# Returning the softmax sums: two wide blocks and three small products in place of three narrow blocks and two transposes

## The chip, the cores and the metric

The kernel runs on one core of a Trainium2 chip. The metric is the device time of one execution in microseconds (us). Lower is better.

## The reference

An attention over 32 heads (batch 4 x 8 heads, 1152 keys, head size 64) is followed by two mixture-of-experts layers over the 2304 resulting rows. The attention pools the queries in pairs, so that there are 576 of them for each head:

```python
q_pool = q.reshape(B, H, S // 2, 2, D).mean(axis=3)
scores = scale * np.matmul(q_pool, k.transpose(0, 1, 3, 2))
scores = scores - np.max(scores, axis=-1, keepdims=True)
attn = np.exp(scores)
attn = attn / (np.sum(attn, axis=-1, keepdims=True) + 1e-09)
return np.matmul(attn, v).astype(np.float32)
```

The change concerns `np.sum(attn, axis=-1)`: one number for each of the 576 queries of a head. The two layers behind it (rows of 512 numbers, 8 experts with hidden size 1024, one expert for each row, the first with a skip decision) are the same before and after.

## The kernel before

**Stages.** The first half of the time is attention, head by head; then the rows, sorted by expert, go through the two layers in tiles of 128. While the attention of a head runs, the numbers by which its rows will be routed are computed too (`back_logits`, `divide`).

**The attention of a head.** Scores stand transposed: keys on the partitions (9 tiles of 128, index `t`), the 576 queries in two halves of 288 columns. For each `t` TensorE makes the scores (L566 and L571, two parts of one product), ScalarE takes the exponent into `P` (L850), and GpSimd adds the nine tiles of `P` up into `Acc`, 128 x 576 (L443, L446). TensorE also makes blocks of scores of the next head (`prior`, L556), which VectorE reduces to row maxima (L1037), and transposes keys and queries of the heads to come (`trans_k`, `trans_qh`, `trans_ql`; all transposes have the line L504).

**The way back of a head.** When head `h` runs, head `h - 1` is finished off. `weighted` (L587) multiplies by the values: the output, 64 partitions for each half of the queries, lies in a PSUM bank as two column blocks of 64, one for each half. `sums` (L600) then multiplies `Acc` by a block of ones, which adds up its 128 partitions; since every column of the stationary block is ones, each block of output partitions holds the same sums. ScalarE copies the outputs to `OT` (L866) and the sums to `ST` (L870). `back_values` transposes `OT` in three pieces of 96 queries, `back_sums` brings the sums of `ST` to the same 96 partitions, `back_logits` multiplies `OT` by the routing weights (L622), and VectorE's `divide` adds 1e-9, takes the reciprocals (L1053) and multiplies.

**Order.** TensorE's order is written out by hand in `body(h)`: for every `t` the scores, two `prior` blocks and then what is listed under `if t == ...`. The values' third group and the sums stand at t = 4, `back_values` and `back_sums` at t = 5, `back_logits` at t = 6. Each engine works through its own list; semaphores join them. `sums` waits for `acc_step` (GpSimd), `back_values` for `ot_out` and `st_out` (ScalarE), `divide` for `out_done` (the last of L622). `body` runs for h = -2 to 32; heads are 0 to 31. PSUM bank `TR` (7) takes transposes and the sums, bank `OB` (6) the outputs, the routing logits and the ranks. In GpSimd's list, some rows are scattered between heads (L460).

The f32 products have two records each in the trace, one for each pass; transposes have one.

Of the kernel before, what the change touches and what calls it, by code (L numbers as in the profile page):

```python
# [5 lines left out]
def attention_moe_moe(nc, q, k, v, w_skip, w_gate1, w1a, w2a, w_gate2, w_ogate, w1b, w2b, out):  # L6
# [11 lines left out]
    ALU, ACT, AX = mybir.AluOpType, mybir.ActivationFunctionType, mybir.AxisListType  # L18
    ds = bass.ds
    PN = 128  # L20


    B, H, S, D = q.shape
    NH = B * H
    SQ = S // 2
    HQ = SQ // 2
# [8 lines left out]
    OP = 96  # L35
    OJ = HQ // OP
# [28 lines left out]
    with ctx:  # L65
        def sb(name, shape, dt=f32):
            return ctx.enter_context(nc.sbuf_tensor(name, shape, dt))

        def sem(name):
            return ctx.enter_context(nc.semaphore(name))  # L70
# [36 lines left out]
        Acc = view["acc"]  # L107
# [2 lines left out]
        QHT = [at(f"QHT{u}", M_K + 4 * (5 * S + u * SQ), [PN, SQ], f32r) for u in range(3)]  # L110
        QLT = [at(f"QLT{u}", M_K + 4 * (5 * S + (3 + u) * SQ), [D + 1, SQ], f32r) for u in range(2)]
        OT = sb("OT", [PN, HQ])
        SG = 3
        SW = SQ // SG
        SR = 32 * (SG - 1) + 1
        SJ = SW // OP
        ST = sb("ST", [SR, SW])
        mx3 = sb("mx3", [PN, QT, NB])
        den = sb("den", [OP, 2 * OJ])
        rden = sb("rden", [OP, 2 * OJ])  # L120
# [4 lines left out]
        ident = sb("ident", [PN, PN])  # L125
        ones = sb("ones", [PN, 64])
# [96 lines left out]

        PS = ctx.enter_context(nc.psum_tensor("PS", [PN, 8, 512], f32))
        MXB, SB, OB, TR = 0, 2, 6, 7
        LOG, RANK, SUMS = 0, 192, 288
        HB, XTB, YB, X1B, LB, RKB = 0, 2, 3, 4, 5, 6


# [17 lines left out]
        sum_done, st_out = sem("sum_done"), sem("st_out")  # L247
        out_done = sem("out_done")
        norm = sem("norm")
# [5 lines left out]
        def wait(eng, s, val):  # L255

            if val > 0:
                eng.wait_ge(s, val)
# [17 lines left out]
        def has(g):  # L276
            return 0 <= g < NH
# [224 lines left out]
        def _(pe):  # L502
            def transpose(o, i, n=PN):
                return nc.tensor.transpose(o, i, ident[0:n, 0:n])  # L504

            def keep_busy(n, bank=OB):

                for _ in range(n):
                    transpose(PS[:, bank, 0:PN], ident[:, :])
# [83 lines left out]
            def sums(g):  # L593

                pe.wait_ge(acc_step, ACCS * (g + 1))
                if has(g + 3):
                    pe.wait_ge(qht_out, 2 * (g + 3) + 2)
                wait(pe, norm, HEAD_NORM * (g - 1) + 4)
                for r in range(SG):
                    last = nc.tensor.matmul(PS[32 * r:32 * r + 32, TR, 0:SW], ones[:, 0:32],  # L600
                                            Acc[g % 2][:, r * SW:(r + 1) * SW], start=True, stop=True)
                last.then_inc(sum_done, 1)

            def back_values(g):

                pe.wait_ge(ot_out, g + 1)
                pe.wait_ge(st_out, g + 1)
                for j in range(OJ):
                    transpose(PS[0:OP, TR, j * PN:(j + 1) * PN], OT[:, j * OP:(j + 1) * OP])

            def back_sums(g):

                for n in range(SJ):
                    transpose(PS[0:OP, OB, SUMS + n * SR:SUMS + (n + 1) * SR], ST[:, n * OP:(n + 1) * OP], SR)

            def back_logits(g):

                if g == 0:
                    pe.wait_ge(wrh_in, 16 * 8)
                for j in range(OJ):  # L620
                    o = LOG + j * 2 * NL
                    last = nc.tensor.matmul(PS[0:OP, OB, o:o + 2 * NL], OT[:, j * OP:(j + 1) * OP],  # L622
                                            wrh[:, g % H].rearrange("p a n -> p (a n)"), start=True, stop=True)
                last.then_inc(out_done, 1)
# [23 lines left out]
            def body(h):  # L648

                now, after, before = has(h), has(h + 1), has(h - 1)  # L650
                blocks = iter(range(NBLK))
                for t in range(KT):
                    if t == 3 and has(h + 2):
                        trans_qh(h + 2, 0)
                    if now:
                        scores(h, t, 0)
                    if after and t < 7:
                        prior(h + 1, next(blocks))
                    if after and t < 7 and h <= 0:
                        keep_busy(1)  # L660
                    if now:
                        scores(h, t, 1)
                    if after and t < 7:
                        prior(h + 1, next(blocks))
                    if after and t < 7 and h <= 0:
                        keep_busy(2 if h < 0 else 1)
                    if t == 0:
                        if has(h + 2):
                            trans_k(h + 2, 0)
                            if h == FIRST:  # L670
                                keep_busy(14)
                        if before:
                            weighted(h - 1, 0)
                    if t == 1 and has(h + 2):
                        trans_k(h + 2, 1)
                        if h == FIRST:
                            keep_busy(5)
                    if t == 2 and before:
                        weighted(h - 1, 1)
                    if t == 3 and has(h + 2):  # L680
                        if h == FIRST:
                            keep_busy(5)
                        trans_qh(h + 2, 1)
                        if h == FIRST:
                            keep_busy(4)
                    if t == 4:
                        if before:
                            weighted(h - 1, 2)
                            sums(h - 1)
                        if after:  # L690
                            prior(h + 1, next(blocks))
                    if t == 5 and before:
                        back_values(h - 1)
                        back_sums(h - 1)
                    if t == 6 and h - 2 in RANKS_IN:
                        ranks_of_batch(RANKS_IN.index(h - 2))
                    if t == 6 and before:
                        back_logits(h - 1)
                    if t == 7 and after:
                        trans_ql(h + 1, 0)  # L700
                        trans_ql(h + 1, 1)
# [73 lines left out]
            for m in range(2):  # L775
                pe.wait_ge(tables[m], 1)
                trans_x(m, 0)
                start = 0
                for e in range(E):
# [15 lines left out]
                    start = end  # L795
# [15 lines left out]
        def _(act):  # L811
# [55 lines left out]

            def s_out(g):
                act.wait_ge(sum_done, g + 1)
                nc.scalar.copy(ST[:, :], PS[0:SR, TR, 0:SW]).then_inc(st_out, 1)  # L870

            def route_exps(b):

# [55 lines left out]
            for m in range(2):  # L929
# [12 lines left out]
                start = 0  # L942
                for e in range(E):
# [27 lines left out]
                    start = end  # L971
# [5 lines left out]
        def _(dve):  # L977
            vec = nc.vector
# [66 lines left out]
            def divide(g):  # L1045

                T = PS[0:OP, TR, 0:OJ * PN].rearrange("p (j a d) -> p j a d", j=OJ, a=2)
                dve.wait_ge(out_done, g + 1)
                total = PS[0:OP, OB, SUMS:SUMS + SJ * SR].rearrange("p (n k) -> p n k", n=SJ)[:, :, 0:SR:32]
                vec.tensor_scalar(den.rearrange("p (r n) -> p r n", n=SJ), total.rearrange("p n r -> p r n"),  # L1050
                                  1e-9, None, ALU.add).then_inc(norm, 1)
                dve.wait_ge(norm, HEAD_NORM * g + 1)
                vec.reciprocal(rden[:, :], den[:, :]).then_inc(norm, 1)  # L1053
                dve.wait_ge(norm, HEAD_NORM * g + 2)
                b, c = g // H, (g % H) * D
                by = rden[:, :].rearrange("p (a j) -> p j a", a=2).unsqueeze(3)
                vec.tensor_tensor(tmpL[:, :, :, :], PS[0:OP, OB, LOG:LOG + OJ * 2 * NL]
                                  .rearrange("p (j a n) -> p j a n", j=OJ, a=2),
                                  by.broadcast_to([OP, OJ, 2, NL]), ALU.mult).then_inc(norm, 1)
                if b >= 2 and g % H == 0:  # L1060
                    dve.wait_ge(rt_scat[b % 2], 16 * TB * (b // 2))
                vec.tensor_tensor(xrow[b % 2][:, :, c:c + D].rearrange("p (a j) d -> p j a d", a=2), T,
                                  by.broadcast_to([OP, OJ, 2, D]), ALU.mult).then_inc(norm, 1)
                dve.wait_ge(norm, HEAD_NORM * g + 3)
                Lb = L[:, b * TB:(b + 1) * TB, :].rearrange("p (a j) n -> p j a n", a=2)
                vec.tensor_tensor(Lb, Lb, tmpL[:, :, :, :], ALU.add).then_inc(norm, 1)
# [197 lines left out]
            for m in range(2):  # L1264
# [12 lines left out]
                start = 0  # L1277
                for e in range(E):
# [28 lines left out]
                    start = end  # L1307
# [28 lines left out]
```

## Time and profile before

| | |
|---|---|
| median of three runs | 1139.82 us (1138.76 to 1144.27) |
| the profiled execution | 1139.82 us |
| its span, first to last instruction | 1138.1 us |
| TensorE matmuls busy | 1093.4 us, 96% |
| VectorE, ScalarE, GpSimd busy | 740.7, 531.8, 452.8 us |
| sums, L600 | 192 matmuls, 338 ns each in the median |
| transposes of `ST` | 64 matmuls, 220 ns each in the median |
| logits, L622 | 192 matmuls, 248 ns each in the median |

How to read it: matmuls overlap, the next starting before the end of the one before, so that their durations don't add up. The distance from start to start is what one of them takes of the engine's time. "PEld" is the load of the stationary operand, which has a record of its own. Shapes such as 128*96 128x50 mean: a stationary operand of 128 partitions and 96 columns, a moving operand of 128 partitions and 50 columns; the moving operand is named first behind the arrow.

### The profile page before, as it was taken

To read this page: it belongs to the slowest core of one execution; us is meant where nothing else is said; L and a number is where in the kernel's file an instruction comes from. 1 tells how busy PE (TensorE), PEld (TensorE's weight loads), DVE (VectorE), ACT (ScalarE), POOL (GpSimd) and SP (SyncE) were. 2 spreads that over 40 slices of the span, in tenths; PEclk is the share of its full clock that TensorE was granted. 3 is DMA by queue.
4 is the path that set the end of the run, shared out by engine and by line. 5 is a ranking of instruction groups with operands and counts; after the bars stand their busy time and mean duration, and the time that the engine had idled before them with its cause. 6 is when DMAs were issued, how large, how long until landed. Compare 5 with 4: busy or idle time off the path is not lost.

```text
span 1138.1 us, 22000 instructions
## 1 busy us (share of the span) xinstructions
PE 1093.4 (96%) x7757; PEld 916.7 (81%) x7757; DVE 740.7 (65%) x1706; ACT 531.8 (47%) x945; POOL 452.8 (40%) x339
## 2 busy tenths in 40 slices
PE   7999999999999999999779999999699999999996
PEld 6777777777777777777578999999589999999995
DVE  7767767887778777785436777676445655555641
ACT  3566655555655555564124444444143434353420
POOL 0768877677877788677600000000000000001000
PEclk8999999999999999999899999999799999999998
DMA  5272225223322233211649014447384281241100
GB/s 130 66 229 74 63 74 147 74 69 92 102 64 73 74 94 93 76 33 39 220 159 366 28 37 177 170 173 273 134 322 132 111 317 54 58 156 37 46 10 15
DMA packets 74397, 132.59 MB, mean 117 GB/s; under 512 B 11040, under 2 KB 29472, under 8 KB 74320
## 3 DMA queue, kind: packets, MB, share of 16 engines
q10 hardware_dynamic: 26240, 69.22, 16.8%
q1 hardware_dynamic: 43424, 50.58, 16.6%
q0 software_dynamic: 4656, 11.79, 3.0%
q8 instruction: 45, 0.74, 0.3%
q14 instruction: 32, 0.26, 0.1%
HBM read 106.12 MB, written 19.24 MB: 110 GB/s over the span
## 4 chain that ended last, share of the span: by engine, by line
PE 86%; DVE 5%; issue 2%; DMA 2%; POOL 2%; ACTq 1%; ACT 1%; SPq 0%; DVEq 0%; POOLq 0%
PE PS L734 20%; PE PS L587 13%; PE PS L556 9%; PE PS L504 8%; PE PS L566 7%; PE PS L571 7%; PE PS L751 6%; PE PS L747 6%; PE PS L748 6%; DVE W2L L1142 2%; PE PS L622 1%; PE PS L600 1%; PE PS L766 1%; POOL arena_a L446 1%; DMA moe<-xs 1%
## 5 line engine op out<-in xcount | busy, mean ns | idle before, releaser
L446 POOL TENSOR_TENSOR arena_a<-arena_a,arena_p 128x576 f32<-128x576 f32 x224 | 332.9, 1486 | 86.6 <-ACT arena_p L850 63.8
L1037 DVE TENSOR_REDUCE mx<-PS 128x1 f32<-128x384 f32 (+1 forms) x480 | 246.8, 551 | 110.6 <-PE PS L556 106.7
L734 PE MATMUL PS<-moe,W 128*128 128x128 f32 x2432 | 281.3, 277 | 1.6 <-ACT moe L936 1.6
L734 PEld LDWEIGHTS PS<-moe,W 128*128 128x128 f32 x2432 | 278.4, 193 | 4.0 <-ACT moe L936 2.2
L850 ACT ACTIVATE arena_p<-PS 128x576 f32<-128x576 f32 x288 | 187.7, 653 | 135.7 <-PE PS L571 135.1
L566 PE MATMUL PS<-QHT,KA 128*128 128x288 f32 x576 | 187.1, 329 | 0.0
L556 PE MATMUL PS<-KA,QHT 128*128 128x384 f32 (+1 forms) x480 | 176.1, 368 | 1.8 <-DVE mx L1037 1.8
L571 PE MATMUL PS<-QLT,KB 65*128 65x288 f32 x576 | 171.3, 301 | 0.3 <-ACT QLT L861 0.3
L822 ACT CAST W2H<-W2R 128x1024 fp32r<-128x1024 f32 x148 | 144.3, 1048 | 52.7 <-PE PS L751 39.7
L1142 DVE TENSOR_TENSOR W2L<-W2R,W2H 128x1024 fp32r<-128x1024 f32 x144 | 166.5, 1219 | 1.4 <-ACT W2H L822 1.4
L587 PE MATMUL PS<-arena_p,arena_a 128*64 128x288 f32 x1152 | 160.5, 414 | 0.0
L494 POOL DMA_INDIRECT out<-moe,oidx x23 | 22.8, 990 | 294.6 <-DVE moe L1302 294.6
L956 ACT ACTIVATE hTh<-PS 128x512 fp32r<-128x512 f32 x76 | 45.2, 596 | 190.5 <-PE PS L734 190.5
L747 PE MATMUL PS<-W2H,hTh 128*128 128x512 f32 x304 | 123.7, 407 | 1.3 <-ACT hTh L956 1.3
L566 PEld LDWEIGHTS PS<-QHT,KA 128*128 128x128 f32 x576 | 109.3, 190 | 16.8 <-issue 14.3
L748 PE MATMUL PS<-W2L,hTh 128*128 128x512 f32 x304 | 119.1, 392 | 0.0
L587 PEld LDWEIGHTS PS<-arena_p,arena_a 128*64 128x64 f32 x1152 | 74.3, 136 | 55.2 <-issue 16.9
L571 PEld LDWEIGHTS PS<-QLT,KB 65*128 65x128 f32 x576 | 109.1, 189 | 5.7 <-issue 5.7
L477 POOL DMA_INDIRECT xs<-moe,tpu x16 | 18.0, 1123 | 225.3 <-DVE tpu L1261 225.3
L556 PEld LDWEIGHTS PS<-KA,QHT 128*128 128x128 f32 (+1 forms) x480 | 86.4, 180 | 21.9 <-DVE mx L1037 9.5
L751 PE MATMUL PS<-W2H,hTl 128*128 128x512 f32 x304 | 82.7, 394 | 3.9 <-DVE hTl L1221 3.9
L504 PE MATMUL PS<-ident,arena_a 128*128 128x128 f32 (+2 forms) x480 | 81.7, 279 | 4.2 <-DVE KA L1023 2.1
(174 smaller groups left out, 1138.8 us busy)
## 6 DMA issues: line engine op xcount, KB each, us to landing
W<-in_moe_w ACTq DMA_DIRECT2D x16, 2048.0 KB, 15.0
W2R<-in_moe_w ACTq DMA_DIRECT2D x16, 2048.0 KB, 9.8
moe<-xs SPq DMA_DIRECT2D x40, 258.0 KB, 2.7
arena_a<-in_k SPq DMA_DIRECT2D x32, 288.0 KB, 2.9
arena_a<-in_v SPq DMA_DIRECT2D x32, 288.0 KB, 2.8
KB<-KA SPq DMA_DIRECT2D x32, 288.0 KB, 3.1
arena_a<-in_q SPq DMA_DIRECT2D x32, 256.0 KB, 3.2
xs<-padrow SPq DMA_DIRECT2D x8, 258.0 KB, 3.3
```

Of the source, the lines that this page charges most:

```text
L446: nc.gpsimd.tensor_tensor(Acc[u], Acc[u], P[u][:, t, :], ALU.add).then_inc(acc_step, 1)
L504: return nc.tensor.transpose(o, i, ident[0:n, 0:n])
L556: nc.tensor.matmul(PS[0:n, MXB + b % 2, 0:KB_], QHT[g % 3][:, t * PN:t * PN + n], KA[g % 3][:, c * KB_:(c + 1) * KB_], start=True, stop=Tr ...
L566: nc.tensor.matmul(o, KA[g % 3][:, t * PN:(t + 1) * PN], QHT[g % 3][:, cols], start=True, stop=False)
L571: last = nc.tensor.matmul(o, KB[u][:, t * PN:(t + 1) * PN], QLT[u][:, cols], start=False, stop=True)
L587: last = nc.tensor.matmul(PS[64 * half:64 * half + D, OB, 0:HQ], Vt[u][:, t, :], P[u][:, t, half * HQ:(half + 1) * HQ], start=(t == 0), st ...
L734: last = nc.tensor.matmul(PS[:, HB + f // 4, (f % 4) * PN:(f % 4 + 1) * PN], W1[s][:, d, f * PN:(f + 1) * PN], xT[:, d, :], start=(d == 0) ...
L747: nc.tensor.matmul(PS[:, YB, 0:DM], hTh[:, f, :], W2H[s][:, f, :], start=(f == 0), stop=False)
L748: nc.tensor.matmul(PS[:, YB, 0:DM], hTh[:, f, :], W2L[s][:, f, :], start=False, stop=False)
L850: nc.scalar.activation(P[u][:, t, :].rearrange("p (a c) -> p a c", a=2), PS[:, b:b + 2, 0:HQ], ACT.Exp, scale=SCALE).then_inc(exp_done, 1)
L1037: vec.reduce_max(mx3[0:n, t, c:c + 1], PS[0:n, MXB + b % 2, 0:KB_], AX.X).then_inc(pr_max, 1)
L1142: ins = vec.tensor_tensor(W2L[s][:, f, :], W2R[s][:, f, :], W2H[s][:, f, :].bitcast(f32), ALU.subtract)
```

## The change

The sums are made by two products with a stationary block of 64 ones and 288 moving columns each, one for each half of the queries, in place of three with a block of 32 ones and 192 columns. So `ST` holds one half's sums in its first 64 partitions and the other's in partition 64 (65 partitions, 288 columns; before 65 and 192, with the three thirds in partitions 0, 32 and 64).

To bring them to the 96 partitions, `ST` is no longer transposed (two transposes of 96 columns, 65 moving columns each, into bank `OB`). It is the stationary operand of three products of 96 columns, and the moving operand is two columns of the identity, 0 and 64, which pick the two partitions: six numbers for each partition, in bank `TR` behind the transposed outputs. These stand in TensorE's list at t = 6, ahead of `back_logits`, and no longer at t = 5. ScalarE copies 288 columns in place of 192, and `divide` reads six adjoining columns and the order of pieces and halves in `den` and `rden` is turned round.

```diff
-        SG = 3
-        SW = SQ // SG
-        SR = 32 * (SG - 1) + 1
-        SJ = SW // OP
-        ST = sb("ST", [SR, SW])
+        SR = D + 1
+        ST = sb("ST", [SR, HQ])
...
-                for r in range(SG):
-                    last = nc.tensor.matmul(PS[32 * r:32 * r + 32, TR, 0:SW], ones[:, 0:32],
-                                            Acc[g % 2][:, r * SW:(r + 1) * SW], start=True, stop=True)
+                for half in range(2):
+                    last = nc.tensor.matmul(PS[64 * half:64 * half + 64, TR, 0:HQ], ones[:, 0:64],
+                                            Acc[g % 2][:, half * HQ:(half + 1) * HQ], start=True, stop=True)
...
-                for n in range(SJ):
-                    transpose(PS[0:OP, OB, SUMS + n * SR:SUMS + (n + 1) * SR], ST[:, n * OP:(n + 1) * OP], SR)
+                for j in range(OJ):
+                    o = OJ * PN + 2 * j
+                    nc.tensor.matmul(PS[0:OP, TR, o:o + 2], ST[:, j * OP:(j + 1) * OP],
+                                     ident[0:SR, 0:SR:SR - 1], start=True, stop=True)
...
                     if t == 5 and before:
                         back_values(h - 1)
-                        back_sums(h - 1)
...
                     if t == 6 and before:
+                        back_sums(h - 1)
                         back_logits(h - 1)
...
-                nc.scalar.copy(ST[:, :], PS[0:SR, TR, 0:SW]).then_inc(st_out, 1)
+                nc.scalar.copy(ST[:, :], PS[0:SR, TR, 0:HQ]).then_inc(st_out, 1)
...
-                total = PS[0:OP, OB, SUMS:SUMS + SJ * SR].rearrange("p (n k) -> p n k", n=SJ)[:, :, 0:SR:32]
-                vec.tensor_scalar(den.rearrange("p (r n) -> p r n", n=SJ), total.rearrange("p n r -> p r n"),
-                                  1e-9, None, ALU.add).then_inc(norm, 1)
+                both = PS[0:OP, TR, OJ * PN:OJ * (PN + 2)]
+                vec.tensor_scalar(den[:, :], both, 1e-9, None, ALU.add).then_inc(norm, 1)
...
-                by = rden[:, :].rearrange("p (a j) -> p j a", a=2).unsqueeze(3)
+                by = rden[:, :].rearrange("p (j a) -> p j a", a=2).unsqueeze(3)
```

## Rows read from the trace of the kernel before

**Rows 1.** The page: span, and each engine's busy time, share and instructions.

```profile
span 1138.1 us, 22000 instructions
...
PE 1093.4 (96%) x7757; PEld 916.7 (81%) x7757; DVE 740.7 (65%) x1706; ACT 531.8 (47%) x945; POOL 452.8 (40%) x339
```

**Rows 2.** Busy time by stretch (us; instructions), granted TensorE clock, DMA share, GB/s.

```profile
37.00:300.00 263.00, 262.80 (x1894) 199.02 (x1894) 191.98 (x434) 156.46 (x310) 202.55 (x136) 1.00 0.36 99
...
316.50:532.00 215.50, 215.50 (x1558) 163.44 (x1558) 166.47 (x380) 122.90 (x246) 159.13 (x110) 1.00 0.27 71
532.00:553.00 21.00, 19.87 (x155) 14.08 (x156) 4.92 (x14) 9.11 (x18) 18.84 (x15) 1.00 0.28 86
553.00:577.60 24.60, 14.31 (x103) 13.22 (x97) 10.96 (x53) 1.39 (x4) 9.36 (x10) 0.72 0.73 266
```

**Rows 3.** Timeline, TensorE, end of one head's values to the next transposes.

```profile
314.23 0.66 PE L587 MATMUL PS<-arena_p,arena_a 128*64 128x288 f32 x4
...
314.47 0.41 PE L587 MATMUL PS<-arena_p,arena_a 128*64 128x288 f32 x2
314.81 0.53 PE L600 MATMUL PS<-arena_a,ones 128*32 128x192 f32 x6
315.27 0.44 PE L556 MATMUL PS<-KA,QHT 128*128 128x384 f32 x1
...
316.59 0.49 PE L504 MATMUL PS<-ident,OT 128*96 128x128 f32 x3
...
317.22 0.29 PE L571 MATMUL PS<-QLT,KB 65*128 65x288 f32 x1
...
319.05 0.71 PE L504 MATMUL PS<-ident,arena_a 128*65 128x128 f32 x5
...
319.73 0.30 PE L571 MATMUL PS<-QLT,KB 65*128 65x288 f32 x1
```

**Rows 4.** Timeline, TensorE: inside one group of logits products (L622).

```profile
318.10 0.50 PE L622 MATMUL PS<-wrh,OT 128*96 128x50 f32 x4
...
318.27 0.33 PE L622 MATMUL PS<-wrh,OT 128*96 128x50 f32 x2
```

**Rows 5.** Timeline, TensorE: 16-column products and the shortest steps, second half.

```profile
622.17 0.60 PE L766 MATMUL PS<-wr,moe 128*128 128x16 f32 x4
622.62 0.48 PE L747 MATMUL PS<-W2H,hTh 128*128 128x512 f32 x1
...
625.47 0.18 PE L772 MATMUL PS<-tRb,trib 128*128 128x16 bf16 x1
625.51 0.17 PE L773 MATMUL PS<-Raccb,onesb 128*128 128x16 bf16 x1
```

**Rows 6.** Weight loads by form (line, stationary shape, count, busy us, mean ns).

```profile
L622 PEld LDWEIGHTS PS<-wrh,OT 128*96 128x96 f32 x192 | 21.2, 166 | 0.3
...
L504 PEld LDWEIGHTS PS<-ident,OT 128*96 128x96 f32 x96 | 11.4, 125 | 1.8 <-issue 0.9
L504 PEld LDWEIGHTS PS<-ident,ST 65*96 65x96 f32 x64 | 7.6, 127 | 0.0
```

**Rows 7.** Timeline, VectorE and ScalarE around the same head.

```profile
321.08 1.02 DVE L1037 TENSOR_REDUCE mx<-PS 128x1 f32<-128x384 f32 x2 [0.34 <-PE PS L556]
...
314.93 0.40 ACT L866 COPY OT<-PS 128x288 f32<-128x288 f32 x1 [1.14 <-PE PS L587]
...
316.46 0.65 ACT L850 ACTIVATE arena_p<-PS 128x576 f32<-128x576 f32 x1 [0.74 <-PE PS L571]
```

**Rows 8.** Timeline, GpSimd in the last two heads, then all engines after it.

```profile
532.10 6.08 POOL L446 TENSOR_TENSOR arena_a<-arena_a,arena_p 128x576 f32<-128x576 f32 x4 [1.45 <-ACT arena_p L850]
...
542.08 10.70 POOL L446 TENSOR_TENSOR arena_a<-arena_a,arena_p 128x576 f32<-128x576 f32 x7
...
552.83 0.53 PE L600 MATMUL PS<-arena_a,ones 128*32 128x192 f32 x6 [1.13 <-POOL arena_a L446]
...
553.41 0.32 ACT L870 COPY ST<-PS 65x192 f32<-65x192 f32 x1 [1.26 <-PE PS L600]
```

More of the change, by code:

```diff
@@ L225, in attention_moe_moe @@
         MXB, SB, OB, TR = 0, 2, 6, 7
-        LOG, RANK, SUMS = 0, 192, 288
+        LOG, RANK = 0, 192
         HB, XTB, YB, X1B, LB, RKB = 0, 2, 3, 4, 5, 6
```

## The prediction

> **What bounds the kernel now.** I read the page's totals first: TensorE's matmul queue is busy for 96% of the span, the next engine, VectorE, for 65% [rows 1]. An average over stages decides nothing, so the busy time by stretch came next. The edit touches only the attention stage, and there TensorE is busy for 262.80 of 263.00 us and for all of a further 215.50 us, at a granted clock of 1.00, its upper level of 2.4 GHz; VectorE, ScalarE and GpSimd each have a fifth or more of the same stretches free [rows 2]. So from 37 to 532 us a nanosecond more or less on TensorE moves everything behind it, and work on another engine counts only where TensorE waits for it. TensorE's timeline was then read step by step, from the start of one group of instructions to the start of the next: a matmul's own duration overlaps that of its neighbour and is no price [rows 3].
>
> In the last stretch before the second part this changes: from 532 to 553 us TensorE is idle for 1.1 us [rows 2]. GpSimd's timeline shows why: its additions start each without a pause behind the one before, until the last sum matmuls, which wait 1.13 us for them [rows 8]. So head 31 ends when GpSimd does, and TensorE's work of head 30's return (done while head 31 runs) is hidden.
>
> **The sums (L600).** Before, three column blocks of 32 run side by side, 192 columns each, in two passes. From the last pair of value matmuls to the matmul behind the sums is 315.27 - 314.47 = 0.80 us: 0.34 us until the sums start, 0.46 us for them [rows 3]. After, they are two column blocks of 64 with 288 columns, which is the exact form of L587. That form's pairs start 0.24 us apart (314.47 - 314.23), and a change of form costs more: 0.34 us from the last pair to the next form [rows 3]. If the sums simply go on as two more pairs of L587's form, the time is 0.24 + 0.24 + 0.34 = 0.82 us: **+0.02 us** for a head. The larger column count is paid for by one change of form less. If the border between the two groups costs a change of form in spite of equal shapes, it is 0.34 + 0.24 + 0.34 = 0.92 us: +0.12 us. I take the first, since shape and place on the array are the same. (The Trainium skill, TensorEngine Tiling (Array Packing), section Key Properties, says that changing the tiling mode drains TensorE and changing only the tile does not; by that rule it is +0.02 us, and without it +0.12 us, and the 0.10 us beyond the pair's own pace at a change of form agrees with it.)
>
> **The sums' way back, removed.** Two transposes of `ST` stood behind the three of `OT`. From the first of those to the L571 behind them is 317.22 - 316.59 = 0.63 us. The five transposes at 319.05, followed by the same L566 and L571, take 319.73 - 319.05 = 0.68 us, and their own pace is 0.11 us each (128 columns, the same as for `OT`), so three alone would take 0.68 - 2 x 0.11 = 0.46 us [rows 3]. Removed: **-0.17 us**.
>
> **The sums' way back, added.** Three f32 products, stationary `ST` 65x96, moving 2 columns. The trace has two records for each f32 product (192 of L622 for 32 heads of three), so six matmuls with six weight loads. None of this form exists before. The nearest row is L622: the same 96 stationary columns, f32, 50 moving columns; its matmuls start 0.17 us apart for two, 0.085 us each [rows 4]. With 128 stationary and only 16 moving columns (L766) the step is longer, (622.62 - 622.17) / 4 = 0.112 us [rows 5]: fewer moving columns and yet slower, so the step follows the weight load and not the moving data. The load's length goes by columns and not rows, for the transposes of 128 and of 65 rows with 96 columns take 125 and 127 ns [rows 6]. So 6 x 0.085 = **+0.51 us**. Bounds: upwards 6 x 0.112 = 0.67 us; downwards the shortest step of two small products, L772 to L773, 0.04 us [rows 5], which is also 0.085 less the 41 ns by which a transpose's weight load is shorter than L622's [rows 6]: 6 x 0.04 = 0.24 us; below that nothing at all, if the six slipped wholly under their neighbours. I take 0.085, the row with the same type and stationary columns. (The Trainium skill, TensorE: Matmul & The Clock Gate, section LDWEIGHTS (loading the stationary operand), puts a load at the column count divided by 1.2 in ns, whatever the rows: 80 ns for 96 columns, six for 0.48 us; the step of 0.085 agrees.)
>
> **What else moves.** The products stand at t = 6 instead of t = 5 and wait for nothing new there. ScalarE's copy into `ST` grows from 192 to 288 columns. The copy of 288 columns beside it takes 0.40 us against its own 0.32 us [rows 7, 8], so +0.08 us, hidden behind the 0.74 us that ScalarE then waits for scores [rows 7]; The copy of `OT` starts at 314.93 and takes 0.40 us, another 0.40 us for `ST` ends it all by about 315.8, and `back_values`, which waits for it, starts at 316.59 [rows 3, 7]. Without that cover it would be 0.08 us a head, 2.6 us in all. VectorE's `divide` can begin some 0.5 us later, behind the longer group; queued behind it are `pool_q` and the next maxima, and VectorE waits 0.34 us for TensorE before those [rows 7]; TensorE itself comes to them some 0.36 us later, so nothing is short. DMAs, GpSimd's queue and SP's are the same.
>
> **The sum.** A head: +0.02 - 0.17 + 0.51 = +0.36 us. The returns of heads 0 to 28 run inside the TensorE-bound stretch: 29 x 0.36 = 10.4 us. Head 29's is done while head 30 runs, up to the border at 532 us: its sums count (+0.02), the products behind are hidden by GpSimd, which works without a pause from 532.10 [rows 8]; head 30's is hidden likewise. Head 31's has no cover: the sums +0.12 us (from 0.53 to 0.24 + 0.41, [rows 3, 8]), the copy +0.08, the way back +0.34, together 0.5 us. In all +11.0 us. The profiled execution took 1139.82 us, of which 1138.1 are the span, and it is the median of the three runs as well: 1139.8 + 11.0 = **1150.8, say 1151 us**.
>
> **Rivals.** What can be told from no change in this kernel is about 0.5%, 5.7 us.
> - Same work, but a change of form at the border of values and sums: 30 x 0.10 = 3 us more, 1154 us. For it: L600 shows 0.34 us there now; against it: its shape differs, the new one's doesn't.
> - The new loads are priced like L766's: 29 x 6 x 0.027 = 4.7 us more, 1156 us. Against it: those have 128 columns.
> - Not slower beyond what can be measured: the six small products step at 0.04 us. Then a head costs +0.02 - 0.17 + 0.24 = +0.09 us, the total is 3 us, 1143 us. For it: the moving data are 2 columns, and L772/L773 do it; against it: those are bf16, and f32 loads hold L622 and L766 back. It decides from the point where a product steps in under 0.055 us (29 x 0.18 + 0.5 = 5.7 us).
> - The added time is absorbed by waits of TensorE in each head: only head 31's 0.5 us stays, 1140 us. Against it: 262.80 of 263.00 us busy.
> - The six products cost nothing: 29 x -0.15 us = -4.3 us, 1136 us, on the edge of faster. It needs a step of zero, which no row has.
>
> **How the numbers follow.** Main case 0.73; change of form 0.10; loads as L766's 0.04; steps of 0.04 us 0.08; absorbed 0.03; free 0.02. Slower by over 0.5% in the first three: 0.87; within 0.5% in the next two: 0.11; faster 0.02. The range must leave out no more than 2 in 10: 1146 to 1157 us holds the first three. Its lower end allows products of 0.06 us; both ends leave some 2 us for the second part, which starts 11 us later in a stretch with the granted clock at 0.72 on average [rows 2], so that the clock may rise at another point of the work. The main case's own range is 1148 to 1154 us.
>
> **What would show it.** In the changed profile: the matmul of the new way back x192, about 0.085 us from start to start, with weight loads of about 166 ns; the sums starting 0.24 us, not 0.34 us, behind the last L587 pair, and 0.82 us from there to L556; 0.46 us from the first `OT` transpose to L571; heads 0.36 us further apart than the present distance; TensorE still without idle time from 37 us to the last two heads; VectorE's wait before the next maxima not grown. The prediction is wrong if the small products step far under 0.085 us, if the border drains, or if `ST` or `den` turns up as something TensorE waits for.

## The result, and the profile after

The changed kernel takes 1151.59 us in the median of five runs (1149.71 to 1152.43), the kernel before 1140.47 us in the same measurement (1138.76 to 1144.27). The ratio is 1.0093, with a 95% interval of 1.0078 to 1.0107: slower by 11.1 us. The forecast was 11.0 us slower, 1151 us. Single executions of one kernel lie up to 5.5 us apart here, so an agreement to 0.1 us in the total says little; the steps below say more.

The totals of the page and three stretches of the changed kernel (us busy for TensorE, its weight loads, VectorE, ScalarE, GpSimd, with instructions; then granted clock, DMA share, GB/s), beside [rows 1, 2]:

```profile
span 1151.4 us, 22128 instructions
...
PE 1108.2 (96%) x7821; PEld 934.3 (81%) x7821; DVE 740.1 (64%) x1706; ACT 534.6 (46%) x945; POOL 454.2 (39%) x339
```

```profile
37.00:300.00 263.00, 262.80 (x1884) 202.41 (x1882) 189.37 (x428) 155.03 (x303) 198.95 (x134) 1.00 0.35 97
300.00:543.00 243.00, 243.00 (x1744) 187.29 (x1742) 182.26 (x417) 136.26 (x271) 177.90 (x123) 1.00 0.28 72
543.00:564.00 21.00, 20.59 (x160) 14.89 (x158) 4.47 (x14) 9.32 (x18) 18.80 (x14) 1.00 0.24 74
```

TensorE is as full as before and gets through fewer of the old instructions: in the first 263 us it does 1884 matmuls in place of 1894, although each head has two more, and every other engine is busy for a little less of the same stretch. That is what a bound engine with more to do looks like; the share of 96% did not move at all. Such a share hides short waits, though. This line of the weight loads of the changed kernel is one of them:

```profile
322.58 0.13 PEld L553 LDWEIGHTS PS<-KA,QHT 128*64 128x64 f32 x1 [0.18 <-DVE mx L1036]
```

The third `prior` block in this stretch waits for a maximum of VectorE, and its start comes 0.23 us behind the one before, where it is 0.14 us a moment earlier (321.90 to 322.04). The kernel before has the same wait at 316.36 us, so it takes nothing from the comparison.

The timeline of TensorE shows the steps. These rows answer to [rows 3, 4] (L584 is the old L587, L597 the old L600, L553 the old L556, L563 the old L566, L568 the old L571, L621 the old L622; L612 is new):

```profile
320.66 0.41 PE L584 MATMUL PS<-arena_p,arena_a 128*64 128x288 f32 x2
320.90 0.66 PE L597 MATMUL PS<-arena_a,ones 128*64 128x288 f32 x4
321.49 0.44 PE L553 MATMUL PS<-KA,QHT 128*128 128x384 f32 x1
...
322.81 0.49 PE L501 MATMUL PS<-ident,OT 128*96 128x128 f32 x3
...
323.27 0.30 PE L568 MATMUL PS<-QLT,KB 65*128 65x288 f32 x1
...
324.03 0.59 PE L612 MATMUL PS<-ident,ST 65*96 65x2 f32 x6
324.06 0.56 PE L612 MATMUL PS<-ident,ST 65*96 65x2 f32 x5
324.48 0.69 PE L621 MATMUL PS<-wrh,OT 128*96 128x50 f32 x6
324.99 0.38 PE L563 MATMUL PS<-QHT,KA 128*128 128x288 f32 x1
325.21 0.29 PE L568 MATMUL PS<-QLT,KB 65*128 65x288 f32 x1
325.34 0.29 PE L563 MATMUL PS<-QHT,KA 128*128 128x288 f32 x1
325.47 0.30 PE L568 MATMUL PS<-QLT,KB 65*128 65x288 f32 x1
```

The line at 324.06 is a closer view of the one above it: the last five of the six. They and the border to L621 are five steps of 0.085 us; the first step is 0.03 us.

The sums start 0.24 us behind the last value pair and no longer 0.34, and from that pair to L553 it is 321.49 - 320.66 = 0.83 us (before 0.80). From the first transpose of `OT` to L568 it is 0.46 us (before 0.63). From the first small product to the instruction behind the logits it is 324.99 - 324.03 = 0.96 us; the logits alone took 0.45 us before (317.97 to 318.42). So +0.03, -0.17 and +0.51: +0.37 us. The trace's median distance from one head's `OT` transposes to the next head's went from 16.53 to 16.91 us, +0.38 us.

The weight loads by form, beside [rows 6] (count, busy us, mean ns): the new load is as long as that of L621, of 128 rows, and not as short as that of a transpose of the same `ST` (127 ns in [rows 6]).

```profile
L612 PEld LDWEIGHTS PS<-ident,ST 65*96 65x96 f32 x192 | 21.0, 164 | 0.3
...
L621 PEld LDWEIGHTS PS<-wrh,OT 128*96 128x96 f32 x192 | 18.9, 165 | 0.0
...
L501 PEld LDWEIGHTS PS<-ident,OT 128*96 128x96 f32 x96 | 11.3, 125 | 1.9 <-issue 1.1
```

The last head's way back, all engines, beside [rows 8]:

```profile
564.08 0.71 PE L597 MATMUL PS<-arena_a,ones 128*64 128x288 f32 x4 [0.49 <-POOL arena_a L443]
...
564.83 0.40 ACT L869 COPY ST<-PS 65x288 f32<-65x288 f32 x1 [0.80 <-PE PS L597]
```

The last sums begin at 564.08 us and no longer at 552.83, 11.25 us later, and TensorE waits 0.49 us for GpSimd there, not 1.13. From the start of the sums to the copy it is 0.75 us in place of 0.58, and the copy takes 0.08 us more.

### The profile page after: what moved, and what is told of

Its sections match the earlier page's. It is cut to its first block, busy times and chain, and to the rows that moved or that the text cites. A ratio compares the mean times of both kernels' runs of the same rounds, so it can differ in the third digit from the quotient of the medians.

```text
span 1151.4 us, 22128 instructions
## 1 busy us (share of the span) xinstructions
PE 1108.2 (96%) x7821; PEld 934.3 (81%) x7821; DVE 740.1 (64%) x1706; ACT 534.6 (46%) x945; POOL 454.2 (39%) x339
## 4 chain that ended last, share of the span: by engine, by line
PE 87%; DVE 5%; issue 2%; DMA 2%; POOL 2%; DVEq 0%; ACT 0%; ACTq 0%; SPq 0%; POOLq 0%
PE PS L733 21%; PE PS L584 13%; PE PS L553 9%; PE PS L501 8%; PE PS L563 7%; PE PS L568 7%; PE PS L750 6%; PE PS L746 6%; PE PS L747 6%; PE PS L621 1%; DVE W2L L1140 1%; PE PS L597 1%; PE PS L765 1%; PE PS L612 1%; POOL arena_a L443 1%
## 5 line engine op out<-in xcount | busy, mean ns | idle before, releaser
L563 PE MATMUL PS<-QHT,KA 128*128 128x288 f32 x576 | 187.0, 329 | 0.0
L553 PE MATMUL PS<-KA,QHT 128*128 128x384 f32 (+1 forms) x480 | 176.2, 368 | 1.8 <-DVE mx L1036 1.8
L568 PE MATMUL PS<-QLT,KB 65*128 65x288 f32 x576 | 171.1, 301 | 0.3 <-ACT QLT L860 0.3
L584 PE MATMUL PS<-arena_p,arena_a 128*64 128x288 f32 x1152 | 160.5, 414 | 0.0
L563 PEld LDWEIGHTS PS<-QHT,KA 128*128 128x128 f32 x576 | 109.4, 190 | 17.0 <-issue 14.5
L584 PEld LDWEIGHTS PS<-arena_p,arena_a 128*64 128x64 f32 x1152 | 74.4, 136 | 55.2 <-issue 16.9
L568 PEld LDWEIGHTS PS<-QLT,KB 65*128 65x128 f32 x576 | 109.1, 189 | 6.0 <-issue 6.0
L553 PEld LDWEIGHTS PS<-KA,QHT 128*128 128x128 f32 (+1 forms) x480 | 86.4, 180 | 25.9 <-issue 13.1
```

What stands on the lines that cost most here:

```text
L553: nc.tensor.matmul(PS[0:n, MXB + b % 2, 0:KB_], QHT[g % 3][:, t * PN:t * PN + n], KA[g % 3][:, c * KB_:(c + 1) * KB_], start=True, stop=Tr ...
L563: nc.tensor.matmul(o, KA[g % 3][:, t * PN:(t + 1) * PN], QHT[g % 3][:, cols], start=True, stop=False)
L568: last = nc.tensor.matmul(o, KB[u][:, t * PN:(t + 1) * PN], QLT[u][:, cols], start=False, stop=True)
L584: last = nc.tensor.matmul(PS[64 * half:64 * half + D, OB, 0:HQ], Vt[u][:, t, :], P[u][:, t, half * HQ:(half + 1) * HQ], start=(t == 0), st ...
```

## The experiments

What each kernel took, and the median distance from head to head in its trace, which is the sharper measure: the changed kernel, e6 and e7, whose TensorE has the same list but for the moved columns, agree in it to 0.002 us. The whole times hold more than the heads. In these traces the first products with the values start anywhere from 39.5 to 42.5 us, before any sums; e3 and e9 start latest (42.47 and 42.31 us), the kernel before and the changed one at 40.38 and 40.53 us. Why is open. "Against before" is the difference from the kernel before in the same measurement.

| kernel | median us | before us | ratio, 95% interval | against before | head to head us |
|---|---|---|---|---|---|
| before | | 1140.47 | | | 16.53 |
| changed | 1151.59 | 1140.47 | 1.0093 (1.0078 to 1.0107) | +11.1 | 16.91 |
| e1_two_blocks_transposed | 1142.67 | 1139.39 | 1.0023 (1.0012 to 1.0034) | +3.3 | 16.61 |
| e2_three_blocks_products | 1144.62 | 1139.39 | 1.0043 (1.0026 to 1.0059) | +5.2 | 16.71 |
| e3_border | 1158.43 | 1139.39 | 1.0159 (1.0140 to 1.0177) | +19.0 | 17.11 |
| e4_again_96 | 1167.39 | 1139.39 | 1.0242 (1.0225 to 1.0259) | +28.0 | 17.42 |
| e5_again_72 | 1164.77 | 1141.06 | 1.0217 (1.0200 to 1.0234) | +23.7 | 17.33 |
| e6_moving_65 | 1151.12 | 1141.06 | 1.0087 (1.0071 to 1.0104) | +10.1 | 16.91 |
| e7_copy_twice | 1151.06 | 1141.06 | 1.0094 (1.0074 to 1.0114) | +10.0 | 16.91 |
| e8_at_t5 | 1151.62 | 1141.06 | 1.0092 (1.0076 to 1.0109) | +10.6 | 16.93 |
| e9_one_pass_sums | 1134.14 | 1140.71 | 0.9942 (0.9926 to 0.9959) | -6.6 | 16.32 |

**The two halves of the change, alone.** First only the sums, with the old kind of return:

```diff
-                for j in range(OJ):
-                    o = OJ * PN + 2 * j
-                    nc.tensor.matmul(PS[0:OP, TR, o:o + 2], ST[:, j * OP:(j + 1) * OP],
-                                     ident[0:SR, 0:SR:SR - 1], start=True, stop=True)
+                for j in range(OJ):
+                    transpose(PS[0:OP, OB, SUMS + j * SR:SUMS + (j + 1) * SR], ST[:, j * OP:(j + 1) * OP], SR)
```

> Only the sums of the change (two blocks of 64 by 288 columns); the way back is by transposes of ST again, now three of 65 moving columns, at t = 5. Theory (the cost of the change lies in the six small products, the wider sums are nearly free): a head costs +0.02 for the sums and +0.06 for one transpose more than before, +0.08 us, so the distance between heads is 16.62 us (before 16.535, changed 16.913) and the time is 2.7 us above before, 1143 us. Rival (the wider sums are the cost, because a change of form is not saved): +0.12 and +0.06, 16.72 us a head and 1146 us; the sums would start 0.34 us behind the last value pair and not 0.24.

16.61 us a head, +0.08 as the theory had it. The rival asked for 16.72 us and a start of the sums 0.34 us behind the last value pair; here too it is 0.24. TensorE's timeline of this kernel:

```profile
315.95 0.66 PE L597 MATMUL PS<-arena_a,ones 128*64 128x288 f32 x4
316.54 0.44 PE L553 MATMUL PS<-KA,QHT 128*128 128x384 f32 x1
...
317.85 0.49 PE L501 MATMUL PS<-ident,OT 128*96 128x128 f32 x3
318.18 0.34 PE L501 MATMUL PS<-ident,ST 65*96 65x65 f32 x3
318.32 0.38 PE L563 MATMUL PS<-QHT,KA 128*128 128x288 f32 x1
```

From the first transpose of `OT` to the L568 behind this stretch it is 0.69 us (317.85 to 318.54), where the changed kernel, with no `ST` there, has 0.46. So three transposes of `ST` cost 0.23 us, for the same data that need 0.51 us as products. So the wider sums are nearly free and the products are the cost.

Then only the products, two of them behind the old sums:

```diff
-                for n in range(SJ):
-                    transpose(PS[0:OP, OB, SUMS + n * SR:SUMS + (n + 1) * SR], ST[:, n * OP:(n + 1) * OP], SR)
+                for n in range(SJ):
+                    o = OJ * PN + SG * n
+                    nc.tensor.matmul(PS[0:OP, TR, o:o + SG], ST[:, n * OP:(n + 1) * OP],
+                                     ident[0:SR, 0:SR:32], start=True, stop=True)
```

> Only the way back of the change: the sums stay three blocks of 32 by 192 columns, and ST comes back by two products of 96 stationary columns that move three columns each, at t = 6. Theory (a product's price is its weight load, 0.085 us for 96 columns, two of them for each f32 product): -0.17 + 4 x 0.085 = +0.17 us a head, 16.71 us, and 29 x 0.17 + 0.2 = 5 us above before, 1145.5 us. Rival (the price is the product's own overhead, paid per product and not per weight load): the step of this kernel would not be 0.085 us.

16.71 us a head, +0.17 (16.706 - 16.533). In its timeline the four products and the six of the logits together take 320.80 - 320.01 = 0.79 us, where the logits alone took 0.45. That is 0.34 us for four steps of 0.085 us, and with the 0.17 us of the transposes taken off it is +0.17. The rival predicted another step, and falls; but two products with four loads can't by themselves tell a price for each load from a price for each product. That is done further down, with 72 columns.

**The price of a product, doubled.** The three products are issued a second time, into six columns that nobody reads:

```diff
                 for j in range(OJ):
+                    o = OJ * (PN + 2) + 2 * j
+                    nc.tensor.matmul(PS[0:96, TR, o:o + 2], ST[:, j * 96:(j + 1) * 96],
+                                     ident[0:SR, 0:SR:SR - 1], start=True, stop=True)
+                for j in range(OJ):
```

> The changed kernel with the three products of ST issued twice, the second time into six other columns of the same bank that nobody reads. Theory (0.085 us for each of six weight loads, on an engine without slack): +0.51 us a head, 17.42 us, and 29 x 0.51 + 0.5 = 15.3 us above the changed kernel, 1167 us. Rival (part of the first six is start and end of the group, or TensorE has waits that take some of it): clearly under 0.4 us a head.

17.42 us a head, +0.505 over the changed kernel, 0.084 us for each of six. The rival, that the first six hold a start and an end of their own, falls.

**Load or moving data.** The added products with 72 stationary columns in place of 96 (the `96` of the diff above becomes `72`; the added results are read by nobody):

> As the doubled products, but the added three have 72 stationary columns in place of 96, the same rows and the same two moving columns; their results are read by nobody. Theory (the step follows the stationary columns): in proportion to 0.085 us for 96 and 0.112 us for 128 columns it is 0.064 us for 72, so 6 x 0.064 = +0.39 us a head over the changed kernel, 17.30 us, and about 11.6 us more, 1163 us. Rival (a fixed price of 0.085 us for a small product, whatever its columns): +0.51 us a head, 17.42 us, 1167 us.

17.33 us a head, +0.42, between the two forecasts (0.39 and 0.51) and nearer to the first. TensorE's timeline of this kernel tells why:

```profile
329.27 0.34 PE L553 MATMUL PS<-KA,QHT 128*64 128x384 f32 x1
329.45 0.49 PE L612 MATMUL PS<-ident,ST 65*72 65x2 f32 x6
329.48 0.46 PE L612 MATMUL PS<-ident,ST 65*72 65x2 f32 x5
329.80 0.65 PE L616 MATMUL PS<-ident,ST 65*96 65x2 f32 x6
330.31 0.69 PE L625 MATMUL PS<-wrh,OT 128*96 128x50 f32 x6
```

The first step of a group is short: its first two loads start at 329.27 and 329.45 us, while L553 is recorded until 329.61. Here the short step falls to the 72-column products (six in 0.35 us, of which five steps of 0.065), and the six of 96 columns behind them now take the full 0.51 us in place of the 0.45 between 324.03 and 324.48 of the changed kernel: 0.35 + 0.06 = 0.41 us. The step itself is 0.065 us for 72 columns (329.48 to 329.80 are five of them), 0.085 for 96, and 0.112 for 128 in the kernel before. The fixed price of a product falls.

All 65 columns of the identity moved in place of two of them:

```diff
-                                     ident[0:SR, 0:SR:SR - 1], start=True, stop=True)
+                                     ident[0:SR, 0:SR], start=True, stop=True)
```

> The changed kernel with 65 moving columns (the whole identity of that size) in place of 2 in each of the three products; results go to bank OB and divide picks the same six numbers. Theory (the weight load bounds the step and the moving data hide under it): the step stays 0.085 us and the distance of heads 16.91 us; at most the last step before L622 grows. Rival (the step is load plus moving data, one behind the other): 65 columns at the pace of the transposes of ST, about 0.06 us, are added to each of six, +0.3 us a head or more, 1161 us.

16.91 us a head, unchanged. Thirty times the moving columns cost nothing, so the moving data hide under the load. In its timeline the two groups together are as long as before, 325.17 - 324.20 = 0.97 us against 0.96:

```profile
324.20 0.65 PE L612 MATMUL PS<-ident,ST 65*96 65x65 f32 x6
324.68 0.66 PE L621 MATMUL PS<-wrh,OT 128*96 128x50 f32 x6
325.17 0.38 PE L563 MATMUL PS<-QHT,KA 128*128 128x288 f32 x1
```

**The border between the values and the sums.** One prior block is put between them:

```diff
                             weighted(h - 1, 2)
-                            sums(h - 1)
                         if after:
                             prior(h + 1, next(blocks))
+                        if before:
+                            sums(h - 1)
```

> The changed kernel with the third prior block of t = 4 between the last value group and the sums, so that products of the values' form and of the sums' form no longer adjoin; no work is added. Theory (a change between column blocks and the whole array costs about 0.10 us more than going on in one form, and the changed kernel saves one such pair): a step of 0.34 us from the values to prior, about 0.29 from prior to the sums and 0.34 behind them, so +0.2 us a head against the changed kernel, 17.1 us a head and 6 us more, 1157.5 us. Rival (shapes that adjoin don't matter, the 0.34 us belongs to the end of an accumulation group): no difference, 16.91 us a head.

17.11 us a head, +0.19 over the changed kernel, for the same work in another order. TensorE's timeline of this kernel:

```profile
325.66 0.41 PE L584 MATMUL PS<-arena_p,arena_a 128*64 128x288 f32 x2
326.00 0.44 PE L553 MATMUL PS<-KA,QHT 128*128 128x384 f32 x1
326.38 0.71 PE L597 MATMUL PS<-arena_a,ones 128*64 128x288 f32 x4
327.01 0.40 PE L563 MATMUL PS<-QHT,KA 128*128 128x288 f32 x1
327.25 0.30 PE L568 MATMUL PS<-QLT,KB 65*128 65x288 f32 x1
...
327.83 0.34 PE L553 MATMUL PS<-KA,QHT 128*64 128x384 f32 x1
328.01 0.49 PE L501 MATMUL PS<-ident,OT 128*96 128x128 f32 x3
```

The step from L553 into the sums is 0.38 us, not the 0.29 of the expectation, and from the last value pair to L568 it is 327.25 - 325.66 = 1.59 us, where the changed kernel's timeline has 1.24 (320.66 to 321.90): one change of form in and one out cost 0.35 us. (The `prior` block in between is an fp32r product and the sums are f32, so the type changes at these borders together with the shape.) The heads are only 0.19 us further apart, because some comes back: from that L568 to the transposes of `OT` it is 0.76 us here and 0.91 in the changed kernel (321.90 to 322.81). There the third L553 waits some 0.1 us for VectorE's maximum of the block before the last; here that block was issued earlier, ahead of the sums, and the wait of 0.18 us in its loads is gone. So the distance of heads came out as expected though both terms were missed: the two changes of form cost 0.35 us and not 0.2, and a wait that the expectation didn't know gave 0.15 us back. The time is 7.9 us above the changed kernel, of which the heads explain 30 x 0.19 = 5.8 us; in the profiled executions, 8.1 us apart, 1.9 us are the later start and 0.3 us lie behind the last sums. The rival falls: equal forms that adjoin save a change of form, and one costs more than the 0.10 us that the border alone shows.

**The cover.** ScalarE copies the sums twice, and TensorE waits for both copies:

```diff
-                nc.scalar.copy(ST[:, :], PS[0:SR, TR, 0:HQ]).then_inc(st_out, 1)
+                nc.scalar.copy(ST[:, :], PS[0:SR, TR, 0:HQ]).then_inc(st_out, 1)
+                act.wait_ge(st_out, 2 * g + 1)
+                nc.scalar.copy(ST[:, :], PS[0:SR, TR, 0:HQ]).then_inc(st_out, 1)
```

> The changed kernel with ScalarE's copy into ST made twice, one behind the other with a wait, 0.4 to 0.5 us more in ScalarE's list in each head. Theory (the copy is hidden, ScalarE waits 0.74 us for scores behind it and TensorE comes for ST later than that): distance of heads unchanged at 16.91 us, and only the last head's 0.5 us is seen, 1152 us. Rival (the longer copy is on the path, which would be part of the cost of the change): up to 0.5 us a head, 1166 us.

16.91 us a head, unchanged. ScalarE's timeline of this kernel: the second copy takes the place of idle time, and the wait for scores behind both is still 0.25 us. The 0.5 us of the last head can't be told in the whole time (1151.06 us in the median, 1150.21 to 1153.57).

```profile
320.58 0.40 ACT L869 COPY ST<-PS 65x288 f32<-65x288 f32 x1
321.01 0.40 ACT L871 COPY ST<-PS 65x288 f32<-65x288 f32 x1
321.65 0.65 ACT L849 ACTIVATE arena_p<-PS 128x576 f32<-128x576 f32 x1 [0.25 <-PE PS L568]
```

**The place.** `back_sums(h - 1)` goes back from t = 6, ahead of `back_logits`, to t = 5, behind `back_values`:

> The changed kernel with its three products at t = 5, behind back_values, where the transposes of ST stood, and not at t = 6. Theory (place costs nothing, TensorE has no slack anywhere): distance of heads 16.91 us and 1151.6 us, within 1.5 us. Rival (behind the transposes they delay a prior block for which VectorE waits, or they take a wait of TensorE that is there already at t = 5): a distance that differs by 0.05 us or more either way.

16.93 us a head, +0.02, and 1151.62 us. The rival's bound of 0.05 us isn't reached either way. In TensorE's timeline of this kernel it is 1.00 us from the first transpose of `OT` to L568 (322.47 to 323.47) and 0.45 us for the logits (324.23 to 324.68), together 1.45 us; in the changed kernel it is 0.46 + 0.96 = 1.42. So the six products add 0.54 us behind the transposes and 0.51 ahead of the logits, and that is the 0.02 us.

**A version that is faster than both.** The experiments say that the sums of the kernel before cost TensorE two passes and two changes of form (values to sums, sums to `prior`), and that transposes are the cheap way back. So, on the kernel before (`AccR` is the memory of `Acc` under the type fp32r, and `onesr` a block of zeros with ones in its columns 64 to 95; the lines that set them up are left out here):

```diff
-                        nc.gpsimd.tensor_tensor(Acc[u], Acc[u], P[u][:, t, :], ALU.add).then_inc(acc_step, 1)
+                        to = AccR[u][:, :] if t == KT - 1 else Acc[u]
+                        nc.gpsimd.tensor_tensor(to, Acc[u], P[u][:, t, :], ALU.add).then_inc(acc_step, 1)
...
-                    last = nc.tensor.matmul(PS[32 * r:32 * r + 32, TR, 0:SW], ones[:, 0:32],
-                                            Acc[g % 2][:, r * SW:(r + 1) * SW], start=True, stop=True)
+                    last = nc.tensor.matmul(PS[0:SR + 1, TR, 0:SW], onesr[:, 64 - 32 * r:65 + SR - 32 * r],
+                                            AccR[g % 2][:, r * SW:(r + 1) * SW], start=(r == 0), stop=(r == SG - 1))
```

> A version meant to be faster than both, built on the kernel before: GpSimd writes its last addition of Acc as fp32r, and the sums are three fp32r products of one pass each over the whole array, 66 output partitions, added up in one PSUM region by stationary blocks that have ones only in the 32 columns of their third; ST, its copy and the two transposes are as before. The sums of the exponents are thereby taken from values rounded to fp32r. Theory (prices by steps on a TensorE without slack): one change of form behind the values (0.34 us) and three steps of 192 columns, about 0.09 us each, 0.61 us in place of 0.80, so -0.19 us a head, 16.35 us, and 29 x 0.19 = 5.5 us less than before, 1135 us. Rival (the weight load of 66 columns or a slow first step eats it): between 0 and -0.1 us a head, 1138 to 1140.5 us.

1134.14 us against 1140.71, ratio 0.9942 (0.9926 to 0.9959), 6.6 us faster than before and about 17 us faster than the change; 16.32 us a head, -0.22 us where -0.19 was expected, and the rival (0 to -0.1) falls. TensorE's timeline of this kernel (L604 are the sums, L560 is the prior block, L570 the old L566):

```profile
311.66 1.68 PE L591 MATMUL PS<-arena_p,arena_a 128*64 128x288 f32 x12
313.26 0.48 PE L604 MATMUL PS<-AccR,onesr 128*66 128x192 f32 x3
313.58 0.36 PE L560 MATMUL PS<-KA,QHT 128*128 128x384 f32 x1
313.78 0.29 PE L570 MATMUL PS<-QHT,KA 128*128 128x288 f32 x1
```

The three sums take 0.32 us in place of 0.46, and the step behind them, from L560 to L570, is 0.20 us; behind the sums of the changed kernel it was 0.28 (321.77 - 321.49 in its timeline), and in the kernel before as well. So the gain of 0.22 us is 0.14 us where 0.19 were expected, and 0.08 us that the expectation didn't have: its total was met partly by luck. The weight loads show the difference behind the sums, first of the changed kernel, then of this one:

```profile
321.49 0.19 PEld L553 LDWEIGHTS PS<-KA,QHT 128*128 128x128 f32 x1 [0.44 <-issue]
321.60 0.19 PEld L563 LDWEIGHTS PS<-QHT,KA 128*128 128x128 f32 x1
```

```profile
313.50 0.19 PEld L560 LDWEIGHTS PS<-KA,QHT 128*128 128x128 f32 x1
313.61 0.19 PEld L570 LDWEIGHTS PS<-QHT,KA 128*128 128x128 f32 x1
```

Behind the column-tiled sums the load of `prior` starts with its matmul (321.49 both); behind the sums on the whole array it starts 0.08 us ahead (313.50 and 313.58). In both kernels the next load follows 0.11 us later and its matmul 0.17 us behind that (321.77 and 313.78), so the 0.08 us of the second step are the lead that the first load had or hadn't. This version has one change of form between the values and `prior`, as the changed kernel has, where the kernel before has two; its own slow second step falls on its first sum, which takes 0.145 us where the other two take 0.087. It changed the number of passes, the type and the use of the array all at once, and no run tells apart what each is worth.

## Why the prediction was right

- **What bounds it.** What was added on TensorE came out in full: doubling the products added 0.505 us where their steps sum to 0.51. It isn't quite true that TensorE has no slack: a wait for VectorE hides in each head, and e3 won it back. The forecast is untouched by it, since both kernels have it.
- **The sums, +0.02 us.** Measured +0.03. The main case, no change of form at the border, holds; the rival with 3 us more falls by the 0.24 us step and by the kernel with a prior block in between.
- **The transposes removed, -0.17 us.** Measured -0.17, 0.63 to 0.46.
- **The products, +0.51 us.** Measured +0.51. The row it was taken from (L622, 0.085 us) had other rows and other moving columns, and neither matters: 65 moving columns in place of 2 change nothing, 72 stationary columns give 0.065. The rival of 0.04 us a step rested on bf16 loads and falls, as does the one of 0.112 us. (The Trainium skill, TensorE: Matmul & The Clock Gate, section LDWEIGHTS (loading the stationary operand), gives the column count over 1.2 in ns: 60, 80 and 107 for 72, 96 and 128 columns. The steps of 65, 85 and 112 agree, each 5 ns longer.)
- **The covers.** The longer copy is hidden, shown by making it twice. That `divide` has room shows in VectorE's timeline of the changed kernel, beside [rows 7]:

```profile
325.21 0.16 DVE L1049 TENSOR_SCALAR den<-PS 96x6 f32<-96x6 f32 x1 [0.20 <-PE PS L621]
...
327.63 1.02 DVE L1036 TENSOR_REDUCE mx<-PS 128x1 f32<-128x384 f32 x2 [0.61 <-PE PS L553]
```

  `divide` now waits 0.20 us for the logits, and VectorE still stands idle for 0.61 us ahead of the next maxima, where it was 0.34. The prediction named a growth of that wait as a sign against itself. It grew and was none: it is VectorE that waits there, for a TensorE that comes later. VectorE's list was not lengthened in any kernel.
- **The last heads.** The last sums came 11.25 us later, where 29 x 0.36 + 0.02 = 10.5 were expected. Of the 0.8 us that are missing there, 0.55 are 0.02 us more a head (16.91 - 16.53 = 0.38 and not 0.36), 0.16 were there before the change could act (the first values start at 40.53 and not 40.38 us), and under 0.1 us is GpSimd's. The cover held: `body(30)` delays TensorE by the full 0.34 us of head 29's way back, and GpSimd's last row of additions still begins just 11.2 us later (551.70 against 540.50). Behind the last sums `den` is written 11.61 us later (566.89 against 555.28), so the last head's own share is 0.36 us, where 0.5 were expected; no experiment singled it out, and the granted clock differs there between the two traces (0.72 from 553 to 577.6 us before, 0.79 from 564 to 588.6 us after).
- **The second part.** The profiled execution of the changed kernel is a long one, 1153.12 us; the median is 1151.59. From the start of the last sums to the end of the span it has 1151.4 - 564.08 = 587.3 us, the kernel before 1138.1 - 552.83 = 585.3. Below is the stretch from 589 to 621 us, first of the changed kernel and then of the one with 65 moving columns, whose heads take the same time and whose span is 1149.9 us:

```profile
589.00:621.00 32.00, 29.59 (x196) 26.56 (x197) 16.53 (x38) 12.86 (x20) 1.13 (x1) 0.89 0.61 218
```

```profile
589.00:621.00 32.00, 28.06 (x203) 25.41 (x204) 17.45 (x46) 13.28 (x22) 1.13 (x1) 1.00 0.65 227
```

  The granted clock is 0.89 on average in the first, part of it at the lower level of 1.2 GHz (from 600 to 612 us it is 0.72, in the other kernel 1.00), and TensorE gets 196 matmuls done in 29.59 us where the other gets 203 done in 28.06 us at 2.4 GHz. Where the clock falls differs between them, and it goes with the 1.5 us between their spans; that it is the whole of it wasn't tested. The allowance of 2 us at both ends of the range was of the right size.
- **What was luck.** The heads cost 0.6 us more than forecast and the last one 0.1 us less, and from the last sums to the end it takes between 585.2 and 587.6 us in the traces kept here. That the medians lie 11.1 us apart where 11.0 were forecast is chance; what the runs bear out is each head's sum, 0.38 us for 0.36, and its three terms.

## What to carry to other kernels

On a bound TensorE, price a small f32 product by the load of its stationary columns (0.065 us for 72, 0.085 for 96), twice because of its two passes: one that moves two columns costs as much as one that moves 65, and a transpose of the same data costs less than half. A group of column-tiled products that stands right behind another of the same tile shape saves a change of form. If a sum over partitions can be made on the whole array in one pass, as in the last version, that is cheaper still, at the price of rounding to fp32r. And read the price from the distance between starts: these small products have durations of 215 ns and steps of 85.

## What the runs showed of the hardware that was not expected

- Behind a change from column-tiled products to products on the whole array two steps are slow and not one: the step at the border (0.34 us) and the first behind it (0.28 us from L553 to L563, against 0.20 us behind the sums on the whole array), because the load at the border isn't taken ahead. The prediction knew of the first alone, which did no harm, as both kernels had the second. In and out together cost 0.35 us.
- A slow second step alone is no sign of a change of form. Behind the small products and the logits, which use the whole array, the first L563 takes 0.22 us (324.99 to 325.21) and the next one 0.13 (325.34 to 325.47); the first of these loads starts 0.03 us ahead of its matmul and no more.
- A group of small products has one short step, its first (0.03 us), whatever its columns. With the 72-column products in front, that step is theirs, and the six of 96 columns behind them pay in full: 0.41 us in place of the 0.39 expected.
- Three one-pass fp32r products of 192 columns take 0.32 us, not the 0.27 expected from steps of 0.09: the first is slower behind the change of form (0.145 us).
